# Mix weights loaded and split inside the attention loop, query loads issued ahead of value loads, constants loaded in two parts

## The reference, cut to what matters

```python
# 1. chunked attention: chunks of 32 queries, keys = 8 memory + 16 left + 32 own + 8 right
scores = scale * np.matmul(q_c, k_full.transpose(0, 1, 3, 2))
scores = scores - np.max(scores, axis=-1, keepdims=True)
a = np.exp(scores)
a = a / (np.sum(a, axis=-1, keepdims=True) + 1e-09)
out[:, :, c_start:c_end] = np.matmul(a, v_full)
# 2. channel mix, x_prev = x shifted by one token
xk = mu_k * x + (1.0 - mu_k) * x_prev
xr = mu_r * x + (1.0 - mu_r) * x_prev
k = np.maximum(xk @ w_k, 0.0)
v = k * k @ w_v
r = 1.0 / (1.0 + np.exp(-(xr @ w_r)))
x = r * v
# 3. eight experts, one per token; a token may keep the expert of the token before
h = np.maximum(x[b, s] @ w1[e], 0.0)
out[b, s] = p[e] * (h @ w2[e])
```

## Time and profile before

| | |
|---|---|
| runs | 531.41 us median of 3 (528.64 to 531.82) |
| profiled execution | 533.26 us, its span 531.5 us |
| PE busy | 440.0 us (83%) |
| DVE, ACT busy | 245.9 us (46%), 212.7 us (40%) |
| attention (tile 0 to the first up product) | 14.8 to 82.9 us |
| mix, 6 pairs | 82.9 to about 270 us |
| granted TensorE clock, mean | 0.919 of full |

### The profile page before, as it was taken

The page is one execution under the profiler, slowest core; times in us unless marked ns, Lnnn a source line. Parts: engine busy times, 40 slices in busy tenths (PEclk is TensorE's granted clock), DMA queues, the critical chain, the costliest instruction groups (busy, mean ns, idle before and its releaser), DMA issues.

```text
span 531.5 us, 10141 instructions
## 1 busy us (share of the span) xinstructions
PE 440.0 (83%) x3759; PEld 366.4 (69%) x3759; DVE 245.9 (46%) x477; ACT 212.7 (40%) x319; POOL 55.3 (10%) x62
## 2 busy tenths in 40 slices
PE   1667628999999999999940069999999999999993
PEld 1545518889898989989830047777777777777772
DVE  2454575653535234354045149222382247464861
ACT  1333474663435253344022038222462245555750
POOL 0000000010100101010003601111111111111110
PEclk9967867999999999999975569999999999999998
DMA  8668442428000000000004779511173128383810
GB/s 302 253 208 294 157 181 86 152 90 309 0 0 0 0 0 0 0 0 1 2 0 158 238 281 406 209 54 40 52 227 136 40 71 253 141 251 132 271 61 10
DMA packets 18313, 67.31 MB, mean 127 GB/s; under 512 B 2734, under 2 KB 2734, under 8 KB 18288
## 3 DMA queue, kind: packets, MB, share of 16 engines
q1 hardware_dynamic: 13104, 50.92, 27.9%
q0 software_dynamic: 4896, 16.05, 8.8%
q10 hardware_dynamic: 288, 0.02, 0.0%
HBM read 55.41 MB, written 12.62 MB: 128 GB/s over the span
## 4 chain that ended last, share of the span: by engine, by line
PE 67%; DMA 14%; issue 7%; DVE 5%; POOL 3%; ACT 2%; SPq 1%; POOLq 0%; DVEq 0%; ACTq 0%
PE PS L530 16%; PE PS L403 12%; PE PS L513 12%; PE PS L435 10%; DMA QK<-tiles 5%; PE PS L419 5%; DMA XR<-grouped_rows 5%; POOL grouped_rows L1107 2%; PE PS L521 2%; PE PS L453 2%; PE PS L504 1%; PE PS L330 1%; PE PS L357 1%; DMA RAW<-wmix 1%; PE PS L343 1%
## 5 line engine op out<-in xcount | busy, mean ns | idle before, releaser
L1022 DVE TENSOR_TENSOR ELO<-ERAW,EHI 128x1024 fp32r<-128x1024 f32 x56 | 66.8, 1219 | 12.9 <-ACT EHI L696 10.3
L696 ACT ACTIVATE EHI<-ERAW 128x1024 fp32r<-128x1024 f32 x56 | 57.4, 1053 | 29.6 <-DMA ERAW<-wexp 20.8
L403 PE MATMUL PS<-XHI,WHI 128*128 128x256 f32 x192 | 56.6, 295 | 1.2 <-DVE WLO L805 1.2
L530 PE MATMUL PS<-EHI,HH 128*128 128x512 f32 x128 | 54.6, 426 | 2.6 <-issue 1.0
L403 PE MATMUL PS<-XHI,WLO 128*128 128x256 f32 x192 | 55.2, 287 | 0.0
L403 PE MATMUL PS<-XLO,WHI 128*128 128x256 f32 x192 | 55.1, 287 | 0.0
L513 PE MATMUL PS<-EHI,XSH 128*128 128x512 f32 x128 | 53.0, 414 | 1.4 <-DVE XSL L1030 1.4
L1043 DVE TENSOR_TENSOR HL<-PS,HH 128x512 fp32r<-128x512 f32 x32 | 22.1, 691 | 66.3 <-ACT HH L716 65.9
L513 PE MATMUL PS<-ELO,XSH 128*128 128x512 f32 x128 | 51.5, 402 | 0.0
L513 PE MATMUL PS<-EHI,XSL 128*128 128x512 f32 x128 | 51.2, 400 | 0.0
L530 PE MATMUL PS<-EHI,HL 128*128 128x512 f32 x128 | 50.6, 395 | 0.0
(11 more groups left out here) (141 smaller groups left out, 774.6 us busy)
## 6 DMA issues: line engine op xcount, KB each, us to landing
ERAW<-wexp SPq DMA_DIRECT2D x56, 512.0 KB, 5.6
QK<-tiles SPq DMA_DIRECT2D x12, 768.0 KB, 5.7
VV<-tiles SPq DMA_DIRECT2D x12, 520.0 KB, 3.9
grouped_rows<-ZR POOLq DMA_DIRECT2D x1, 5140.0 KB, 18.1
RAW<-wmix SPq DMA_DIRECT2D x10, 512.0 KB, 3.8
XR<-grouped_rows POOLq DMA_DIRECT2D x17, 257.0 KB, 4.2
CO<-consts SPq DMA_DIRECT2D x1, 470.0 KB, 6.5
rows_out<-OSB,OIDX POOLq DMA_INDIRECT x16, 3.9
```

Of the source, the lines that this page charges most:

```text
L403: last = nc.tensor.matmul(PS[q % 2][:, half * 256:half * 256 + 256], w[:, c:c + P], x[:, k, :], start=n == 0, stop=n == 11)
L530: last = nc.tensor.matmul(PS[4][:, :], x[:, f, :], ww[:, c:c + D], start=n == 0, stop=n == 23)
L696: nc.scalar.activation(EHI[w][:, c * CH2:(c + 1) * CH2], ERAW[c][:], ACT.Copy).then_inc(ehi_done, 1)
L1022: nc.vector.tensor_tensor(ELO[w][:, c * CH2:(c + 1) * CH2], ERAW[c][:], EHI[w][:, c * CH2:(c + 1) * CH2].bitcast(F32), ALU.subtract).then_ ...
```

## The change

Four edits in the code, three in effect. (1) SP loads only the first 128 columns of the constants (the identity) at the start; the other 812 columns are loaded behind the last RAW load, with a semaphore tables_in of their own, for which PE waits ahead of the routing and DVE ahead of the copy of the token numbers, which moves into the first mix pair. (2) `ahead` issues qk_load(t+4) as soon as the scores of tile t+2 are done, then v_load(t+2) when the values product of tile t is done, and then raw_load(t). (3) The RAW loads move into the attention loop, one per tile; a raw_load(n) waits for the WLO of chunk n-2. wlo_done starts at 2, so all later waits count 2 more. (4) ACT and DVE split chunk t-2 in tile t, from tile 2 on, behind exps(t+2) and normed(t); the last pair splits one chunk per tile, and the first mix pair none.

```diff
-            sp.dma_start(CO[:], consts).then_inc(const_in, 16)
+            sp.dma_start(CO[:, 0:C_LT], consts[:, 0:C_LT]).then_inc(const_in, 16)
...
-            def ahead(t, u, more=True):
-
+            def raw_next(n, u):
+
+                sp.wait_ge(wlo_done, n + 1)
+                raw_load(n, u)
+
+            def ahead(t, u):
+
+                sp.wait_ge(scores_done, t + 3)
+                qk_load(t + 4, u)
                 sp.wait_ge(pv_done, t + 1)
                 v_load(t + 2, u)
-                if more:
-                    sp.wait_ge(scores_done, t + 3)
-                    qk_load(t + 4, u)
+                raw_next(t, u)
...
-            ahead(NT - 4, 0, False)
-            ahead(NT - 3, 1, False)
-            for n in range(N1):
-                if n >= 2:
-                    sp.wait_ge(wlo_done, n - 1)
-                raw_load(n, n % 2)
+            for u in range(2):
+                sp.wait_ge(pv_done, NT - 3 + u)
+                v_load(NT - 2 + u, u)
+                raw_next(N1 - 2 + u, u)
+            sp.dma_start(CO[:, C_LT:CW], consts[:, C_LT:CW]).then_inc(tables_in, 16)
...
-            pe.wait_ge(wlo_done, N1A)
+            pe.wait_ge(wlo_done, N1A + 2)
...
+            pe.wait_ge(tables_in, 16)
             pe.wait_ge(route_step, R_FLAGS)
...
-            def weight_hi(n):
-                act.wait_ge(raw_loaded[n % 2], 16 * (n // 2 + 1))
-                nc.scalar.activation(WHI[:, n * CH1:(n + 1) * CH1], RAW[n % 2][:],
+            def weight_hi(n, u):
+                act.wait_ge(const_in, 48)
+                act.wait_ge(raw_loaded[u], 8 * (n - u) + 16)
+                nc.scalar.activation(WHI[:, ds(n * CH1, CH1)], RAW[u][:],
                                      ACT.Copy).then_inc(whi_done, 1)
...
-                    if last:
-                        for n in (2 * u, 2 * u + 1):
-                            weight_hi(n)
+                    if not first:
+                        weight_hi(t - 2, u)
...
                 for q in range(1, 4):
-                    if first:
-                        weight_hi(N1A + q - 1)
                     relu_square(g, q, first)
-                if first:
-                    for n in range(N1A + 3, N1):
-                        weight_hi(n)
...
-                    if last:
-                        for n in (2 * u, 2 * u + 1):
-                            weight_lo(n)
+                    if not first:
+                        weight_lo(t - 2, u)
...
-            nc.vector.tensor_copy(X2R[:, :, D + 1], CO[:, C_TOK:C_TOK + NT])
...
             dve.wait_ge(setup_done, 1)
+            dve.sem_inc(wlo_done, 2)
...
                 squared(g, 2, first)
                 if first:
-                    weight_lo(N1A + 2)
+                    dve.wait_ge(tables_in, 16)
+                    nc.vector.tensor_copy(X2R[:, :, D + 1], CO[:, C_TOK:C_TOK + NT])
                 squared(g, 3, first)
-                if first:
-                    for n in range(N1A + 3, N1):
-                        weight_lo(n)
```

More of the change, by code:

```diff
@@ L35 @@
 QW, KW, VWT = HP * P, HP * CPT * KEYS, HP * CPT * VW
-INW = QW + KW + VWT
+QKW = QW + KW
+INW = QKW + VWT
 NPAIR = NT // 2
@@ L120, in moe_program @@
         inner = top[0]
-        QK = [place(f"QK{i}", [P, QW + KW]) for i in range(2)]
+        QK = [place(f"QK{i}", [P, QKW]) for i in range(2)]
         VV = [place(f"VV{i}", [P, VWT]) for i in range(2)]
@@ L157, in moe_program @@
         const_in = sem("const_in")
+        tables_in = sem("tables_in")
         qk_loaded = [sem(f"qk_loaded{i}") for i in range(2)]
@@ L245, in qk_load @@
             def qk_load(t, u):
-                sp.dma_start(QK[u][:], tiles[ds(t, 1), :, 0:QW + KW].rearrange("a p n -> (a p) n")
+                sp.dma_start(QK[u][:], tiles[ds(t, 1), :, 0:QKW].rearrange("a p n -> (a p) n")
                              ).then_inc(qk_loaded[u], 16)
             def v_load(t, u):
-                sp.dma_start(VV[u][:], tiles[ds(t, 1), :, QW + KW:INW].rearrange("a p n -> (a p) n")
+                sp.dma_start(VV[u][:], tiles[ds(t, 1), :, QKW:INW].rearrange("a p n -> (a p) n")
                              ).then_inc(v_loaded[u], 16)
@@ L410, in gate @@
                 if first:
-                    pe.wait_ge(wlo_done, N1A + KT * D // CH1)
+                    pe.wait_ge(wlo_done, N1A + KT * D // CH1 + 2)
                 else:
@@ L431, in down @@
                     if first and c % CH1 == 0:
-                        pe.wait_ge(wlo_done, c // CH1 + 1)
+                        pe.wait_ge(wlo_done, c // CH1 + 3)
                     r = slice(u * P, u * P + P)
@@ L800, in normed, with weight_lo @@
                 last.then_inc(norm_done, 1)
-            def weight_lo(n):
+            def weight_lo(n, u):
+                dve.wait_ge(const_in, 48)
                 dve.wait_ge(whi_done, n + 1)
-                c = slice(n * CH1, (n + 1) * CH1)
-                nc.vector.tensor_tensor(WLO[:, c], RAW[n % 2][:], WHI[:, c].bitcast(F32),
+                nc.vector.tensor_tensor(WLO[:, ds(n * CH1, CH1)], RAW[u][:], WHI[:, ds(n * CH1, CH1)].bitcast(F32),
                                         ALU.subtract).then_inc(wlo_done, 1)
@@ L881, in mix @@
                     logits_out(2 * g - 2)
-                if first:
-                    weight_lo(N1A)
                 squared(g, 1, first)
@@ L886, in mix @@
                     logits_out(2 * g - 1)
-                else:
-                    weight_lo(N1A + 1)
                 squared(g, 2, first)
                 if first:
-                    weight_lo(N1A + 2)
+                    dve.wait_ge(tables_in, 16)
+                    nc.vector.tensor_copy(X2R[:, :, D + 1], CO[:, C_TOK:C_TOK + NT])
                 squared(g, 3, first)
-                if first:
-                    for n in range(N1A + 3, N1):
-                        weight_lo(n)
                 if not last:
```

## The result

The changed kernel takes 528.31 us (median of 20 runs, 526.46 to 529.85) against 531.68 us before (20 runs, 528.64 to 533.6): a ratio of 0.9942, interval 0.9927 to 0.9958. That is 3.1 us (2.2 to 3.9) where 9.7 were forecast, and above the range of 517 to 527. A second measurement of the same kernel gave 0.9961 (0.9936 to 0.9985).

What follows compares the result with a forecast made beforehand. The attention loop was taken as bound by loads' time to landing, not bandwidth. Savings of 8.05 + 0.4 + 1.2 = 9.7 us brought the profiled 533.26 to 523.6 us, 521.7 as a median; range 517 to 527.

Steps and rivals of the forecast that it cites:

- Part 1: At the start, 406 of 470 KB of constants leave the line: 1.0 us earlier, tile 0 at 13.8.
- Part 2: Attention loop, queries issued ahead of values: tile 2 at 21.8 against 23.64; alone, two tiles from 10.2 to about 8 us.
- Part 3 (a): Attention loop, bytes with a weight load per tile: 1.84 MB at 404 GB/s bound the tile period at 4.56 us.
- the circle (b): Attention loop, DVE and ACT waiting for each other through maxima, exps and splits: 4.84 us per tile, the largest bound.
- The rival of the rate: Attention loop, three mixed streams carry no more than about 355 GB/s: 5.2 us a tile, 524.2 us total; chance 0.16.
- Part 3 (c): Attention loop, SP's query load stands behind a weight load waiting for a split: 4.2 us a tile.
- Slower: Attention loop, late splits block SP and delay queries: 7.2 us a tile, 538.2 us total; chance 0.06.
- The end of attention: Last tiles: mix scalings start at 63.3 instead of 71.35, 8.05 us; 0.4 more without the fourth WLO wait.
- First mix pair: First mix pair: six splits leave, PE's waits of 0.57 and 0.66 go, 1.2 us; the low clock stays.

Runs made afterwards that it cites:

- constants and order: Kernel before with constants in two parts and queries issued ahead of values, weights still behind attention: 527.18 us (0.9929), again 527.10 us (0.9955).
- the fastest kernel: Constants and order, with the first two mix weight chunks loaded at the start and split in the first pair: 521.80 us, 0.9859 of before.

## Why the prediction was wrong

By its own steps:

- **Part 1**, 1.0 us: right. 1.2 in the trace, 0.9 alone.
- **Part 2**, tile 2 at 21.8: measured 22.50, though tile 0 came 0.2 us earlier than forecast, and PE waits for VV there. The sum let both loads run from 16.0 us; V goes out at 16.84, when the values of tile 0 are done. "Alone 8 us for two tiles" was short too: 9.2 (2 x 4.61), since V2 and later V loads are late behind QK. Its 3.0 us were forecast as mostly spent; with the constants they are all of the gain that the experiments show.
- **Part 3 (a), the bytes: this step failed.** The prediction let 1.84 MB a tile move at 404 GB/s, 4.56 us, so the loads bound nothing and cost nothing beyond the circle (b), 4.84. The changed kernel takes 5.51 and 5.20 us a tile. Eight loads without a split cost 4.7 us by themselves. Three other kernels with a full load per tile take 5.09 (no splits), 5.24 (four value buffers) and 5.48 (values first). The start and the loop of the changed kernel, 3 to 13 and 20 to 60 us:

```profile
3.00:13.00 10.00, 2.34 (x128) 1.92 (x128) 3.76 (x14) 2.43 (x3) 0.00 (x0) 1.00 1.01 396
...
20.00:60.00 40.00, 26.91 (x959) 20.58 (x952) 25.73 (x70) 18.09 (x28) 0.00 (x0) 0.71 0.91 330
```

  and the same stretch of the kernel before:

```profile
20.00:60.00 40.00, 26.15 (x1020) 20.22 (x1019) 21.06 (x72) 13.56 (x23) 0.00 (x0) 0.79 0.76 272
```

  With a full load per tile the DMA engines are busy 89 to 96% and carry 326 (values first) to 353 GB/s (no splits). The 404 GB/s came from 3 us with three loads in line. But 330 is a mean, not a rate that the loop runs at. Two parts of it in the changed kernel:

```profile
18.00:30.00 12.00, 6.95 (x269) 5.29 (x270) 7.02 (x21) 5.04 (x9) 0.00 (x0) 0.86 1.01 392
30.00:39.00 9.00, 6.13 (x207) 4.62 (x206) 5.59 (x17) 3.52 (x6) 0.00 (x0) 0.62 0.76 227
```

  The rival of the rate had the size, 5.2 us a tile, chance 0.16, in part by luck, since no fixed rate of 355 shows. The page that it cites (the Trainium skill, DMA: Bandwidth & Descriptors, Bandwidth) gives some 358 GB/s from HBM per core, which makes an estimated 5.15 us. The same section says that this is the share of a core while both cores of a pair stream. It is no limit here: one core runs, and the traces have 396 GB/s over 10 us and 392 over 12.

  The period from tile 2 to tile 10 also holds the stall in the scores of tile 3 and a last tile that waits for no query load. Without the two, from tile 4 to tile 9:

| kernel | us a tile | granted clock | DMA share | GB/s |
|---|---|---|---|---|
| before | 5.21 | 0.76 | 0.72 | 265 |
| changed, two traces | 5.49, 5.53 | 0.69, 0.70 | 0.92, 0.92 | 328, 330 |
| constants and order, two traces | 4.39, 4.17 | 0.81, 0.81 | 0.86, 0.84 | 287, 298 |
| the same with loads, no splits | 5.00 | 0.82 | 0.98 | 359 |
| the same with half the load | 4.69 | 0.78 | 0.95 | 324 |
| the same with splits, no loads | 4.74 | 0.78 | 0.85 | 275 |
| four value buffers | 5.07 | 0.75 | 0.93 | 341 |

  The first and last tile of this stretch in the changed kernel, then the windows of the changed kernel, of loads only and of splits only:

```profile
34.84 1.09 PE L349 MATMUL PS<-CO,PR 128*128 128x128 f32 x4 [0.45 <-ACT PR L577]
...
62.27 1.08 PE L349 MATMUL PS<-CO,PR 128*128 128x128 f32 x4 [2.15 <-DMA VV<-tiles]
```

```profile
34.84:62.27 27.43, 18.86 (x681) 14.56 (x681) 20.65 (x54) 14.31 (x21) 0.00 (x0) 0.69 0.92 328
```

```profile
34.84:59.82 24.98, 17.16 (x681) 13.43 (x681) 14.00 (x48) 8.90 (x15) 0.00 (x0) 0.82 0.98 359
```

```profile
31.02:54.72 23.70, 17.47 (x681) 13.68 (x681) 18.78 (x50) 13.30 (x21) 0.00 (x0) 0.78 0.85 275
```

  Loads alone keep the DMA engines busy 98% of the time at 5.00 us: there the bytes are all but the bound. Why that stretch carries 359 GB/s, where the one from 18 to 30 us carried 392, wasn't tested. The changed kernel takes half a microsecond more although its DMA engines are idle 8% of the time, so the bytes are most of its loss against constants and order, and the last half microsecond is open. Two candidates stand, neither tested. One is SP's order, below. The other is PE's clock: PE is busy 3.8 us a tile at a granted clock of 0.69, and 3.4 at 0.82. Since PE also waits more in the slower kernel, the low clock may be a consequence.
- **Part 3 (b), the circle, 4.84: right in size, not the bound.** For two tiles of the changed kernel DVE's maxima are 4.74 us apart, with nothing idle ahead of the last two:

```profile
48.52 0.75 DVE L767 TENSOR_REDUCE MX<-PS 128x4 f32<-128x256 f32 x2
...
53.26 0.75 DVE L767 TENSOR_REDUCE MX<-PS 128x4 f32<-128x256 f32 x2
...
57.99 0.76 DVE L767 TENSOR_REDUCE MX<-PS 128x4 f32<-128x256 f32 x2
```

  The kernel with splits and no loads takes the same 4.74 from tile 4 to 9, though PE waits for VV there too, so no run shows the circle as the only bound. By the ratios eight splits cost 1.0 us, which isn't clear of noise.
- **Part 3 (c), SP's order: incomplete.** I followed qk_load(t+5) through its waits, and not v_load(t+2), which the change puts behind the queries, with 6.1 us median to landing where it was 3.9. Its own circle, 4.3 of PE + 0.2 + 6.9 of landing (the median from 24 to 56 us) for two tiles, is 5.7 each. Four buffers take this wait away and the whole time stays, so it wasn't the main cause, but it was a term to write down. The slack of over 0.5 us a tile that the prediction saw in SP's order isn't there either. Between 20 and 60 us SP stands waiting for a split ahead of a weight load:

```profile
SPq L256 <- DVE WLO L807: 14.2, 6, 3.1
```

  Three query loads, at 38.28, 49.64 and 54.04 us, go out right behind such a wait, 1.2 to 1.3 us after the end of the scores that free their buffer. In the kernel with loads and no splits SP waits 5.8 us for DVE. This is the mechanism of the rival "Slower", at a small part of its size. No run takes the weight loads off SP's queue, so what it costs isn't shown.
- **The end of attention**: right in kind. 3.5 us of ACT's time went (forecast 3.4), 0.4 behind it (0.4). The scalings started at 70.18 and not 63.3. With the 3.62 us measured from tile 10 to the scalings, 63.3 puts tile 10 at 59.7 and the period from tile 2 at 4.74. So 6.2 of the 6.9 us are the eight tiles, at 5.51 instead of 4.74: 2.9 of them between tiles 2 and 4, the stall of 2.54 included, 3.7 between 4 and 9, and 0.4 back in the last.
- **First mix pair**, 1.2 forecast, 1.8 measured: both waits went, and the first up products were quicker. The first quarter of up took 4.61 us to ACT's first KR (81.30 to 85.91), against 5.11 before. The granted clock was again 0.50 of full, 1.2 GHz, from 78 to 84 us, behind 5.4 idle us of PE:

```profile
78.00:84.00 6.00, 3.85 (x19) 3.44 (x17) 2.32 (x6) 0.79 (x2) 0.00 (x0) 0.50 0.01 3
```

The sum: the loop mis-sized by 6.2 us, a shortfall of 0.7 ahead of it, and 0.6 to the good in the mix pair: 9.7 - 6.2 - 0.7 + 0.6 = 3.4 at the second mix pair, and 3.1 in the ratio. That loads cost the loop time, and how much, is shown by experiment; why the changed kernel loses half a microsecond a tile beyond that, and what the stall is, are open.

## What to carry to other kernels

Before work is moved into a loop that waits for loads, divide all bytes of one turn by a rate that the loop itself sustained over many turns, not by the best 3 us of a trace. Here full loads carried 326 to 353 GB/s over 40 us, with some idle time of the DMA engines in it. The loop before "waited for landing" at 272 GB/s and took 40% more bytes, but not for nothing. Ask too what each new wait in the issuer's queue holds up behind it. When the period changes little and only the load that PE waits for changes, as with four value buffers, more buffers are not the remedy. Move a transfer to where the line is empty (here two loads issued by 10 us), and judge the engine work separately: eight loads cost 4.7 us in the loop, eight splits about 1.0, which isn't clear of noise.

## What the runs showed of the hardware beside that

In every kernel but one with the queries issued first, PE lost 0.8 to 3.0 us once, ahead of the last three of the 64 score matmuls in tile 3, the second tile of the loop's first turn, waiting for nothing that the profile shows:

```profile
31.80 0.42 PE L336 MATMUL PS<-QK 64*32 64x64 f32 x3 [2.54 <-issue]
```

It is absent before, with the constants alone and with the values first, and in the exception, the fastest kernel, whose tile 3 starts at 27.65. The place in the program is always the same, and the instruction queue moves 0.02 MB between 28 and 30 us in this trace, so a late fetch of PE's instructions on a busy line is a candidate. It wasn't tested, and the kernel before moves as much between 28 and 34 us without a stall. It happens once, so at most 0.8 to 3.0 us of the time hang on it. In the changed kernel it lies inside the eight tiles whose period the prediction had wrong, and how much of it the late loads would have cost anyway isn't known.
